# Attention terms earlier on GpSimd, first y ahead of K's transposes, near entries at level 5, x moved by two queues

## The chip, the cores and the metric

The kernel runs on one core of one Trainium2 chip. The metric is the device time of one execution in microseconds. The core has five engines that run their own instruction streams and meet at semaphores: TensorE (PE, matmuls and transposes), VectorE (DVE), ScalarE (ACT), GpSimd (POOL) and SyncE (SP), which here issues all transfers.

## The reference

Three layers in a row. The first is a gated linear attention over 768 time steps, 4 batches and 8 heads of 48 features; then a gated layer and an ELU layer on the 3072 tokens of 384 features.

```python
for t in range(S):
    cur = np.einsum('bhd,bhe->bhde', u[None] * kt, vt)
    y[:, :, t] = np.einsum('bhd,bhde->bhe', rt, state + cur)
    state = wt[:, :, :, None] * state + np.einsum('bhd,bhe->bhde', kt, vt)
...
gate = 1.0 / (1.0 + np.exp(-(x @ w_gate)));  val = x @ w_val
x = gate * val @ w_out
...
h = x @ w_in
g = np.where(h > 0.0, h, np.exp(np.minimum(h, 0.0)) - 1.0)
return g @ w_out
```

w_gate, w_val and w_out of the gated layer are (384, 1536), (384, 1536) and (1536, 384); the last layer's are (384, 2048) and (2048, 384).

## The kernel before

Time is cut into six blocks of 128 steps, each block into two halves of two batches: twelve half blocks, q = 0 to 11. For each, attention runs through the stages Tw, Tk, Tr (TensorE transposes w, k, r; ScalarE copies them out of PSUM), the levels L1 to L6, KT, Y and S, each stage in two parts b = 0 and 1 (one batch each).

The matrix A of scores between steps of a block is built by levels: at level li, runs of L = 2^li steps are paired. VectorE multiplies the later half of each pair of R by decays (`next_level_r`, L875; L879 at the last level), GpSimd the earlier half of K (`next_level_k`, L520), TensorE multiplies the two (L601, L607), and the result goes into A, by VectorE's predicated copies at L1 to L3 (L910), by ScalarE's copies at L4 to L6. The decays of all levels are products of neighbours (L952), made during the transposes by the table `DECAYS`.

The entries of A on the diagonal and one below it, the near entries, come from the untransposed inputs in `nat` (places 0, 1, 2 for r, k, w) and `shift` (r one step later): GpSimd multiplies r'k into `shift` (L498, at L1), rk into k's place of `nat` (L503, at L2) and that by u (L510, at L3); VectorE sums over features at L4 (L917, L921), combines the sums into `near` at L5, and at KT copies `near` into A under a mask (L937). Y multiplies A by V (L621) and adds the old state's part (L627); ScalarE copies it to yT, and SyncE moves it as ten transfers into xs, the input of the gated layer (`move_y`, L380). S updates the state. V, `nat` and `shift` of the next half block are loaded as ten transfers (`load_half`, L328; `load_v`, L349; `load_shift`, L339), once VectorE's sum over rk (d_shift) has freed `nat`.

The gated layer runs over seven sets of tokens: two of 256 columns (half blocks 0 and 1), then five of 512. A set is a list of groups, gate (g), value (v) and output (o) for each of 12 slices of w_gate, w_val and w_out, each in thirds. All products are made from high and low parts: ScalarE writes xh, hh and the weights' high parts, VectorE subtracts to get xl (L958), hl (L962) and the weights' low parts (L983); VectorE also makes h = sig * value (L973). The 36 pieces of these weights are loaded through a ring of four slots (`load_w1`; each load waits until the slot's last piece is split) and split in the first set, the first six ahead of it, in the steps of the list `EARLY`. Piece x = 12 is the first that is loaded after set 0 has begun.

`PROGRAM` is one list of steps, which TensorE, ScalarE and VectorE all walk in this order: half block 0 alone, then each set's thirds with the attention steps of later half blocks spread between them by shares. Set 0 runs beside half block 1, set 1 beside 2 and 3, and sets 2 to 5 beside pairs of half blocks, an even and an odd one; the last set and the ELU layer run without attention. SyncE and GpSimd have orders of their own: SyncE's is written out in its block, GpSimd walks the attention steps alone.

## Time and profile before

| | us |
|---|---|
| median of 3 runs | 1151.97 |
| the runs | 1151.76, 1151.97, 1169.11 |
| the profiled execution | 1157.96 |
| its span | 1156.2 |

| engine | busy us | share of the span |
|---|---|---|
| TensorE, matmuls | 1076.0 | 93% |
| TensorE, weight loads | 928.4 | 80% |
| VectorE | 630.5 | 55% |
| ScalarE | 482.9 | 42% |
| GpSimd | 255.5 | 22% |

The span is that of the profiled execution from the first instruction to the last; its time also holds what lies around it, 1.8 us. All times of instructions are from the start of the span. "L875" is a line of the kernel. In a row of the timeline, the bracket gives how long the engine had been idle and what ended that; a row with x2 or more merges instructions that followed each other.

### The profile page before, as it was taken

The page shows a single profiled execution, that of the slowest core. Times are in us where ns is not written, and L with a number is a line of the kernel's source. Part 1 is how long each engine was busy: PE and PEld are TensorE (multiplying, and loading weights), DVE is VectorE, ACT ScalarE, POOL GpSimd, SP SyncE. Part 2 cuts the span into 40 slices and gives each one's busy share as a digit, 9 for nine tenths or more (in the row PEclk, how much of TensorE's full clock was granted, in tenths as well). Part 3 has the DMA queues.
Part 4 walks back from the last instruction along what each step waited for, and adds up shares of the span by engine and source line. Part 5 has one row for each costly group of instructions (what it writes and reads, how often), then busy time and mean ns, then how long its engine had stood idle before and what let it go on. Part 6 is the DMA issues. An engine that isn't in the chain of part 4 may idle for free.

```text
span 1156.2 us, 19950 instructions
## 1 busy us (share of the span) xinstructions
PE 1076.0 (93%) x8124; PEld 928.4 (80%) x8124; DVE 630.5 (55%) x914; ACT 482.9 (42%) x871; POOL 255.5 (22%) x258
## 2 busy tenths in 40 slices
PE   5576798899999999999999999999999999999998
PEld 4576788877787778778777888889999998999998
DVE  6576778584939484947585633353434333343433
ACT  2434533434343334333433333464545444454543
POOL 8232155151606151524243300000000000000000
PEclk9888999999999999999999999999999999999999
DMA  6527130513413141404130041120101001010000
GB/s 123 104 64 141 51 63 16 90 21 56 63 42 41 37 63 42 59 18 62 42 62 15 9 143 55 55 83 1 55 1 56 1 17 39 1 55 1 28 1 28
DMA packets 154331, 54.97 MB, mean 48 GB/s; under 512 B 115968, under 2 KB 151936, under 8 KB 154240
## 3 DMA queue, kind: packets, MB, share of 16 engines
q1 hardware_dynamic: 154240, 53.70, 21.8%
q8 instruction: 65, 1.06, 0.4%
...
## 4 chain that ended last, share of the span: by engine, by line
PE 72%; DVE 15%; issue 5%; ACT 4%; SPq 2%; DMA 1%; DVEq 0%; ACTq 0%
PE ps L661 19%; PE ps L694 18%; PE ps L686 17%; PE ps L670 8%; DVE RKW L875 6%; DVE A L910 4%; PE ps L586 3%; ACT RKW L715 2%; PE ps L601 2%; PE ps L621 2%; PE ps L627 2%; DVE work L973 1%; DVE hl L962 1%; ACT hh L715 1%; SPq L380 1%
## 5 line engine op out<-in xcount | busy, mean ns | idle before, releaser
L661 PE MATMUL ps<-xh,WS 128*128 128x512 f32 (+1 forms) x1008 | 253.6, 371 | 16.4 <-DVE xl L958 12.0
L715 ACT ACTIVATE hh<-work 128x512 fp32r<-128x512 f32 (+1 forms) x180 | 108.8, 605 | 294.4 <-DVE work L973 209.7
L661 PEld LDWEIGHTS ps<-xh,WS 128*128 128x128 f32 x1008 | 173.4, 192 | 46.5 <-issue 7.3
L694 PE MATMUL ps<-WS,hh 128*128 128x384 f32 x768 | 197.7, 338 | 0.6 <-DVE hl L962 0.6
L670 PE MATMUL ps<-hh,WS 128*128 128x512 f32 (+1 forms) x504 | 162.0, 376 | 19.9 <-DVE hl L962 19.9
L962 DVE TENSOR_TENSOR hl<-work,hh 128x512 fp32r<-128x512 f32 (+1 forms) x180 | 125.6, 698 | 98.9 <-ACT hh L715 98.2
L686 PE MATMUL ps<-xh,WS 128*128 128x512 f32 x576 | 163.3, 396 | 0.0
L520 POOL TENSOR_TENSOR RKW<-RKW,WL 128x256 f32<-128x256 f32 x144 | 124.8, 880 | 158.2 <-PE ps L601 131.6
L1000 DVE SCALAR_TENSOR_TENSOR work<-work,ps 128x512 f32<-128x512 f32 x96 | 66.1, 688 | 168.2 <-ACT work L823 168.2
L694 PEld LDWEIGHTS ps<-WS,hh 128*128 128x128 f32 x768 | 140.7, 188 | 8.1 <-DVE hl L962 1.1
L661 PE MATMUL ps<-xl,WS 128*128 128x512 f32 (+1 forms) x504 | 133.0, 373 | 0.0
L694 PE MATMUL ps<-WS,hl 128*128 128x384 f32 x384 | 129.7, 338 | 0.0
L670 PEld LDWEIGHTS ps<-hh,WS 128*128 128x128 f32 x504 | 93.9, 193 | 38.5 <-DVE hl L962 23.4
L686 PEld LDWEIGHTS ps<-xh,WS 128*128 128x128 f32 x576 | 107.5, 189 | 18.2
L875 DVE TENSOR_TENSOR RKW<-RKW,WL 128x512 f32<-128x512 f32 x120 | 115.7, 982 | 5.7 <-PE ps L601 5.5
L601 PEld LDWEIGHTS ps<-RKW 128*64 128x64 f32 x1920 | 68.4, 145 | 50.1 <-DVE RKW L875 37.9
L601 PE MATMUL ps<-RKW 128*64 128x64 f32 x1920 | 81.4, 236 | 27.3 <-DVE RKW L875 26.5
L821 ACT ACTIVATE work<-ps 128x512 f32<-128x512 f32 x96 | 57.1, 595 | 111.9 <-PE ps L686 111.9
L661 PEld LDWEIGHTS ps<-xl,WS 128*128 128x128 f32 x504 | 86.4, 192 | 13.3
L670 PE MATMUL ps<-hl,WS 128*128 128x512 f32 (+1 forms) x252 | 91.7, 364 | 0.0
L973 DVE TENSOR_TENSOR work<-work,ps 128x512 f32<-128x512 f32 (+1 forms) x84 | 51.2, 609 | 73.0 <-PE ps L661 54.8
L781 ACT ACTIVATE work<-ps 128x512 f32<-128x512 f32 (+1 forms) x84 | 45.1, 537 | 105.0 <-PE ps L661 103.2
...
## 6 DMA issues: line engine op xcount, KB each, us to landing
...
```

The lines of the kernel that those rows point to most:

```text
L520: gp.tensor_tensor(Kb[:, :, :, 0, :], Kb[:, :, :, 0, :], Wb[:, :, :, 1].to_broadcast([P, PR, P // (2 * L), L]), ALU.mult).then_inc(p_k, 1)
L601: last = mm(bank[own, g * C:(g + 1) * C].rearrange("p (e i l) -> p e i l", e=2, l=L), K[:, g, own], Rb[:, :, :, 1, :], start=True, stop=True)
L661: last = mm(ps[:, VAL if val else GATE, t], gate_w(a, val, j, c), xp[b][:, c, t], start=(i == 0 and c == 0), stop=(i == 2 and c == KC - 1))
L670: last = mm(ps[:, ACC + i, t], down_w(a, j, i), hp[b][:, j % 2, t], start=(j == 0 and at == 0), stop=(j == F1 - 1 and at == 2))
L686: last = mm(ps[:, UP2 + j % 4, :], up2_w(a, j, c), xp[b][:, c, :], start=(i == 0 and c == 0), stop=(i == 2 and c == KC - 1))
L694: last = mm(ps[:, ACC2 + b, 0:HD], hp[ap][:, j % 2, b * P:(b + 1) * P], down2_w(wp, j), start=(j == 0 and i == 0), stop=(j == F2 - 1 and i ...
L715: return nc.scalar.activation(o, i, ACT.Copy)
L821: nc.scalar.activation(sig, ps[:, UP2 + j % 4, :], ACT.Relu, scale=-1.0).then_inc(a_relu, 1)
L875: last = tt(Rb, Rb, Wb.unsqueeze(1).unsqueeze(3).to_broadcast([P, 2, n, L]), ALU.mult)
L962: tt(hl[:, j % 2, t], h[:, t], f32(hh[:, j % 2, t]), ALU.subtract).then_inc(d_lo, 1)
L973: tt(h[:, t], sig[:, t], ps[:, VAL, t], ALU.mult).then_inc(d_h, 1)
L1000: nc.vector.scalar_tensor_tensor(h, sig, -1.0, ps[:, UP2 + j % 4, :], ALU.add, ALU.max).then_inc(d_elu, 1)
```

## The change

Five edits. GpSimd's products r'k and rk move from L1 and L2 to Tw, and u's from L3 to Tk; rk is written into w's place of `nat`, so it waits for Tw's transposes (half block 0 keeps the old places in the order). VectorE's sums move from L4 to Tk and Tr, the last decays from Tr to Tk; with the sum over rk at Tr, the loads of the next half block are freed there, and SyncE's order is changed accordingly. The near entries are copied into A at L5, for 32 partitions and 32 columns at a time, in place of KT. In half block 0 Y comes ahead of KT and S, and the six early w1 splits go to KT, S and the next Tw. The ten transfers of the first y are issued half by SyncE, half by ScalarE, and four w1 loads that stood ahead of them now stand behind.

```diff
+    FIRST = STAGES[:-3] + ["Y", "KT", "S"]
+    PARTS = [[("a", q, name, b) for name in (FIRST if q == 0 else STAGES) for b in range(U)] for q in range(NQ)]
...
-    EARLY = [("a", 0, name, b) for name in ("L5", "L6", "KT") for b in range(U)]
+    EARLY = [("a", q, name, b) for q, name in ((0, "KT"), (0, "S"), (1, "Tw")) for b in range(U)]
...
+                if q > 0:
+                    sp.wait_ge(s_att, count("a", q - 1, "Tr", 1))
                 wait(sp, d_shift, q)
...
+                for head in range(0, H, 2 if q == 0 else 1):
+                    for dst, src in y_pieces(q, head):
+                        sp.dma_start(dst, src).then_inc(xs_loaded, 16)
...
             load_shift(1)
+            move_y(0)
             load_w1(NR1 + ONCE, 2 * NR1 + ONCE)
-            move_y(0)
-            at = min(N1, NR1 + split_until(("a", 1, "L4", 1)))
-            load_w1(2 * NR1 + ONCE, at)
             load_half(2)
             load_v(2)
             load_shift(2)
-            load_w1(at, N1)
+            load_w1(2 * NR1 + ONCE, N1)
             move_y(1)
...
-                    if phase["a", q, "L4", 1] == m and q + 1 < NQ:
+                    if phase["a", q, "Tr", 1] == m and q + 1 < NQ:
...
                 elif part == "rk":
                     pool.wait_ge(nat_loaded[0], 32 * (q + 1))
-                    pool.wait_ge(p_shift, q + 1)
-                    gp.tensor_tensor(own, own, heads(nat[:, 0]), ALU.mult).then_inc(p_diag, 1)
+                    pool.wait_ge(nat_loaded[1], 32 * (q + 1))
+                    pool.wait_ge(s_att, count("a", q, "Tw", 1))
+                    gp.tensor_tensor(dest, own, heads(nat[:, 0]), ALU.mult).then_inc(p_diag, 1)
...
-            TERMS = {("L1", 1): "r'k", ("L2", 1): "rk", ("L3", 1): "u"}
+            FIRST_TERMS = {("L1", 1): ["r'k"], ("L2", 1): ["rk"], ("L3", 1): ["u"]}
+            TERMS = {("Tw", 1): ["r'k", "rk"], ("Tk", 0): ["u"]}
...
-                    pe.wait_ge(d_diag, 2 * q + b + 1)
+                    pe.wait_ge(d_diag, 4 * (q + 1))
...
                     copy(yT[:, b, :], ps[:, bank_of("a", q, name, b), :]).then_inc(a_y, 1)
+                    if q == 0 and b == 1:
+                        act.wait_ge(a_y, 2)
+                        for head in range(1, H, 2):
+                            for dst, src in y_pieces(q, head):
+                                nc.scalar.dma_start(dst, src).then_inc(xs_loaded, 16)
...
-            DECAYS = {("Tw", 1): [0], ("Tk", 0): [1], ("Tk", 1): [2, 3], ("Tr", 0): [4, 5, 6]}
+            DECAYS = {("Tw", 1): [0], ("Tk", 0): [1, 2, 3], ("Tk", 1): [4, 5, 6]}
...
+                    if name == f"L{NM + 1}" and b == 1:
+                        dve.wait_ge(a_score, (NL - NM) * q + 1)
+                        dve.wait_ge(d_mask, masked(q, NM - 1))
+                        dve.wait_ge(d_near, 2 * (q + 1))
+                        C = HP // 2
+                        for c in range(P // C):
+                            own, half = slice(c * C, (c + 1) * C), slice(c * C // 2, (c + 1) * C // 2)
+                            nc.vector.copy_predicated(
+                                A[own, :, :, own].rearrange("p g e (i j) -> p (g e) i j", j=2),
+                                masks[own, 0, half].bitcast(I32).unsqueeze(1).unsqueeze(3).to_broadcast([C, 2 * G, C // 2, 2]),
+                                near[own].unsqueeze(2).to_broadcast([C, 2 * G, C // 2, 2])).then_inc(d_diag, 1)
...
+                if (name, b) == (("L4", 0) if q == 0 else ("Tk", 1)):
+                    dve.wait_ge(p_shift, q + 1)
+                    nc.vector.reduce_sum(dots[:, :, 2], shift[:].rearrange("p g e d -> p (g e) d"), axis=AX.X
+                                         ).then_inc(d_dots, 1)
+                elif (name, b) == (("L4", 1) if q == 0 else ("Tr", 1)):
+                    dve.wait_ge(p_diag, 2 * (q + 1))
+                    nc.vector.reduce_sum(dots[:, :, 1], nat[:, 2].rearrange("p g (e d) -> p (g e) d", e=2)[:, :, 0:D],
+                                         axis=AX.X).then_inc(d_shift, 1)
```

VectorE from half block 0's last levels to the split of x. Before: WS rows are w1 low halves, L879 the last level's products, L937 the near copies, L947 the state's sum, L952 the decays, L958 xl.

```order
30 L983 TENSOR_TENSOR WS<-work,WS 128x384
31 L879 TENSOR_TENSOR RKW<-RKW,WL 64x4x64 x2
32 L983 TENSOR_TENSOR WS<-work,WS 128x384
33 L879 TENSOR_TENSOR RKW<-RKW,WL 64x4x64 x2
34 L983 TENSOR_TENSOR WS<-work,WS 128x384
35 L937 COPY_PREDICATED A<-masks,near 128x1024
36 L983 TENSOR_TENSOR WS<-work,WS 128x384
37 L937 COPY_PREDICATED A<-masks,near 128x1024
38 L983 TENSOR_TENSOR WS<-work,WS 128x384
39 L947 TENSOR_TENSOR ST<-SW,ps 48x8x48 x2
```

The same place in the change (line numbers are those of the changed kernel: L930 the near copies, L886 the last level's products, L994 w1 low halves, L950 the state's sum, L955 decays, L958 now the sum over shift, L969 xl):

```order
28 L930 COPY_PREDICATED A<-masks,near 32x16x32 x4
29 L886 TENSOR_TENSOR RKW<-RKW,WL 64x4x64 x4
30 L994 TENSOR_TENSOR WS<-work,WS 128x384 x3
31 L950 TENSOR_TENSOR ST<-SW,ps 48x8x48 x2
32 L994 TENSOR_TENSOR WS<-work,WS 128x384 x2
33 L955 TENSOR_TENSOR WL<-RKW 128x512
34 L994 TENSOR_TENSOR WS<-work,WS 128x384
...
40 L955 TENSOR_TENSOR WL<-WL 128x8
41 L958 TENSOR_REDUCE dots<-shift 128x16
42 L969 TENSOR_TENSOR xl<-xs,xh 128x256 x3
```

The near copies have gone ahead of the last level, the w1 low halves behind it and among the next half block's decays, and all seven decays and a sum now stand ahead of xl.

SyncE after the loads of half block 1. Before: four w1 loads, then the ten transfers of y to xs.

```order
19 L339 DMA shift<-in_r_dram 64x8x48 x2
20 L363 DMA work<-in_moe_w_out_dram 128x384
21 L359 DMA work<-in_moe_w_gate_dram 128x3x128
22 L359 DMA work<-in_moe_w_val_dram 128x3x128
23 L363 DMA work<-in_moe_w_out_dram 128x384
24 L380 DMA xs<-yT 48x2x128 x2
```

In the change (L388 the transfers of y, L371 and L375 w1 loads, L340 the loads of half block 2):

```order
19 L351 DMA shift<-in_r_dram 64x8x48 x2
20 L388 DMA xs<-yT 48x2x128
21 L388 DMA xs<-yT 32x2x128
22 L388 DMA xs<-yT 16x2x128
23 L388 DMA xs<-yT 48x2x128 x2
24 L375 DMA work<-in_moe_w_out_dram 128x384
25 L371 DMA work<-in_moe_w_gate_dram 128x3x128
26 L371 DMA work<-in_moe_w_val_dram 128x3x128
27 L375 DMA work<-in_moe_w_out_dram 128x384
28 L340 DMA nat<-in_w_dram 128x8x48 x2
```

Half of y's transfers are left, they stand ahead of the four w1 loads, and the loads of half block 2 follow right behind those, where 15 more w1 loads stood ahead of them.

GpSimd from the end of half block 1 on. Before (L538 the decayed state, L520 K's products):

```order
36 L538 TENSOR_TENSOR SW<-ST,WL 64x384 x2
37 L520 TENSOR_TENSOR RKW<-RKW 128x256 x2
38 L520 TENSOR_TENSOR RKW<-RKW,WL 128x128x2 x2
39 L498 TENSOR_TENSOR shift<-shift,nat 128x768
40 L520 TENSOR_TENSOR RKW<-RKW,WL 128x64x4 x2
41 L503 TENSOR_TENSOR nat<-nat 128x16x48
42 L520 TENSOR_TENSOR RKW<-RKW,WL 128x32x8 x2
43 L510 TENSOR_TENSOR nat<-nat,ub 128x8x48 x2
```

In the change (L540 and L522 for the same):

```order
37 L540 TENSOR_TENSOR SW<-ST,WL 64x384 x2
38 L498 TENSOR_TENSOR shift<-shift,nat 128x768
39 L503 TENSOR_TENSOR nat<-nat 128x16x48
40 L522 TENSOR_TENSOR RKW<-RKW 128x256
41 L510 TENSOR_TENSOR nat<-nat,ub 128x8x48 x2
42 L522 TENSOR_TENSOR RKW<-RKW 128x256
43 L522 TENSOR_TENSOR RKW<-RKW,WL 128x128x2 x2
```

r'k and rk are ahead of K's first product, u between its two parts, and the levels follow without them.

## Rows read from the trace of the kernel before

**Rows 1.** Busy time by stretch, all engines: stretch, busy, clock granted, DMA share, GB/s.
```profile
core 0: us, PE busy (x) PEld busy (x) DVE busy (x) ACT busy (x) POOL busy (x), PEclk, DMA share, GB/s
0.00:54.00 54.00, 29.32 (x336) 25.06 (x336) 35.34 (x57) 19.94 (x39) 31.47 (x40) 0.95 0.65 121
54.00:128.00 74.00, 55.14 (x579) 52.23 (x579) 49.18 (x82) 30.15 (x70) 18.04 (x18) 0.85 0.40 90
128.00:224.00 96.00, 81.19 (x1017) 75.41 (x1016) 70.95 (x110) 39.51 (x89) 40.22 (x40) 0.96 0.31 54
224.00:1156.00 932.00, 910.32 (x6196) 775.73 (x6196) 475.06 (x666) 393.25 (x674) 165.78 (x160) 1.00 0.17 39
```

**Rows 2.** Timeline, VectorE's near copy and TensorE's Y of half block 0.
```profile
37.13 1.29 DVE L937 COPY_PREDICATED A<-masks,near 128x1024 f32<-128x1024 int32 x1
...
38.57 1.95 PE L621 MATMUL ps<-A,V 128*48 128x128 f32 x16 [3.13 <-DVE A L937]
```

**Rows 3.** Timeline, from y's transfers to the first dense matmul.
```profile
44.45 6.54 SPq L380 DMA_DIRECT2D xs<-yT  x10
...
52.85 1.10 DVE L958 TENSOR_TENSOR xl<-xs,xh 128x256 fp32r<-128x256 f32 x3 [3.75 <-ACT xh L715]
...
54.10 0.98 PE L661 MATMUL ps<-xh,WS 128*128 128x256 f32 x3 [7.13 <-DVE xl L958]
```

**Rows 4.** Waits of TensorE, 54 to 128 us: total, times, longest.
```profile
PE ps L670 <- DVE hl L962: 14.0, 3, 6.5
...
PE ps L661 <- DVE WS L983: 2.3, 2, 1.2
```

**Rows 5.** Timeline, SyncE, ScalarE and TensorE about the longest wait.
```profile
98.50 0.99 SPq L328 DMA_DIRECT2D nat<-in_w_dram  x2
...
108.94 0.62 SPq L359 DMA_DIRECT2D work<-in_moe_w_gate_dram  x1
...
112.07 0.52 ACT L715 ACTIVATE WS<-work 128x384 fp32r<-128x384 f32 x1 [6.79 <-DMA work<-in_moe_w_gate_dram]
...
113.57 0.58 PE L670 MATMUL ps<-hh,WS 128*128 128x256 f32 x1 [6.47 <-DVE hl L962]
```

**Rows 6.** Timeline, VectorE and GpSimd at L1 and L2 of half block 1.
```profile
64.86 2.60 DVE L910 COPY_PREDICATED A<-masks,ps 64x512 f32<-64x512 int32 x2
...
74.83 1.00 DVE L983 TENSOR_TENSOR WS<-work,WS 128x384 fp32r<-128x384 f32 x1 [0.90 <-ACT WS L715]
...
75.38 2.20 POOL L503 TENSOR_TENSOR nat<-nat 128x768 f32<-128x768 f32 x1
...
75.76 2.96 DVE L875 TENSOR_TENSOR RKW<-RKW,WL 128x512 f32<-128x512 f32 x2
...
78.65 1.40 DVE L910 COPY_PREDICATED A<-masks,ps 64x512 f32<-64x512 int32 x2
```

**Rows 7.** One line, VectorE's level products: ns min, median, max, first and last start.
```profile
L875 DVE TENSOR_TENSOR RKW<-RKW,WL x120: 674/714/2361, 14.4 to 644.0; 128x512 f32<-128x512 f32 x120
```

**Rows 8.** Timeline of TensorE, gaps in a steady pair (L5 even, L1 odd).
```profile
479.58 0.69 PE L601 MATMUL ps<-RKW 128*64 128x64 f32 x16 [0.78 <-DVE RKW L875]
...
513.79 0.69 PE L601 MATMUL ps<-RKW 128*64 128x64 f32 x16 [1.94 <-DVE RKW L875]
```

**Rows 9.** Waits of TensorE, 128 to 224 us: total, times, longest.
```profile
PE ps L601 <- DVE RKW L875: 3.0, 7, 0.8
```

**Rows 10.** Timeline behind L5 and L6 of an even half block.
```profile
374.51 1.21 DVE L962 TENSOR_TENSOR hl<-work,hh 128x512 fp32r<-128x512 f32 x1
...
377.74 0.39 PE L670 MATMUL ps<-hh,WS 128*128 128x512 f32 x1
```

**Rows 11.** Timeline of TensorE, second part of Tw and L1, even half block.
```profile
450.37 0.60 PE L586 MATMUL ps<-ident,nat 128*128 128x128 f32 x4
...
459.62 1.39 PE L601 MATMUL ps<-RKW 128*64 128x64 f32 x32
```

**Rows 12.** Groups of GpSimd by form: count, busy us, mean ns, idle before.
```profile
L510 POOL TENSOR_TENSOR nat<-nat,ub 128x384 f32<-128x384 f32 x24 | 29.3, 1242 | 0.0
L503 POOL TENSOR_TENSOR nat<-nat 128x768 f32<-128x768 f32 x12 | 26.7, 2229 | 0.0
```

47 lines of the change are left out of this document (13 added, 34 removed).

## The prediction

> **What bounds the kernel now.** I read first the busy time by stretch [rows 1]. TensorE is idle for 24.7 us of the first 54, for 18.9 of the next 74, 14.8 of the next 96 and 21.7 of the 932 after that. From 630 us on attention is over and TensorE works without gaps; nothing in the change touches that part, so what it can win lies before. Then I asked the timeline what TensorE waited for at each gap, and looked at that engine in the same stretch.
>
> *Before 54 us* everything hangs on the first half block (q=0). The near entries are written into A by two predicated copies at KT, the first from 37.13 us, and Y starts at 38.57 after 3.13 us of waiting [rows 2]. From 44.45 SyncE issues ten transfers of y one after the other, 6.54 us, ScalarE and VectorE split x, and the first dense product starts at 54.10, after 7.13 us of idleness [rows 3].
>
> *54 to 128 us*: three waits for hl take 14.0 us, two for a low half of w1 2.3 [rows 4]. The longest is 6.47 us at 113.57. SyncE, which had waited for the rk sum at L4, issues the ten loads of the next half block from 98.50 to 108.90, and only then the next w1 piece, whose split starts at 112.07 [rows 5]; the two waits for a low half stand before and behind the same jam. The other two waits for hl (7.5 together), and one of 2.0 for h, follow level products of VectorE's that overlap GpSimd's: at L2 a pair takes 2.96 us while GpSimd's rk product of 2.20 runs [rows 6], where the median of one is 0.71 and the longest 2.36 [rows 7]. At L1 and L3 the pairs take 2.92 and 2.57.
>
> *224 to 630 us*: TensorE is idle for 17.9 us, nearly all of it in level matmuls (L601) that wait for VectorE's R product, in one pattern for each of the four pairs of half blocks: four waits in the even one, the last of them 0.78, 2.37 us together; one of 1.94 in the odd one [rows 8].
>
> **Part 1, the first half block: +1.5 us.** Without w1 splits in L5 and L6, VectorE ends L5's second product at about 31.8, and the near copies follow at once. Their form (32 partitions, 512 elements) isn't in the trace. Nearest are L2's copies of 512 elements at 0.70 each (1.40 for two) and L1's at 1.30 (2.60 for two) [rows 6]; by elements the old near copy, 1024 in 1.29 [rows 2], gives 0.65. I take 0.70, as all but L1's agree: four are 2.8 us, to 34.6; bounds 2.6 and 5.2. Y then starts at about 34.7 against 38.57, and yT is ready 3.9 us earlier, at 40.6. The ten transfers are shared: five on SyncE at 0.65 are 3.3 us, issued by 43.9; before they were by 50.99. That is 7 us on paper, and I count none of it, since ScalarE and VectorE aren't free then. The trace has no transfer issued by ScalarE: its price lies between nothing and, by SyncE's, 0.65; I take 0.65. ScalarE is then held until 43.9, and still has ahead of x the six evacuations of KT, Tw and Tk (0.60 each) and six w1 splits (0.52, as at 112.07 [rows 5]): 6.7 us, to 50.6. VectorE follows it with six low halves (0.55), the state's sum (1.14), seven decays (2.3) and, new here, the sum over shift (0.94): 7.7 us from 45.0, to 52.7. With S's matmuls and Tw's transposes, which both wait for ScalarE, I come to 53.6, and xl (1.10) ends at 54.7. GpSimd's rk and u products run in this stretch too, and hold VectorE's products beside them; I add 1 us, less than the 1.5 that the pair at 75.76 lost. So the first dense product starts at about 55.6: what the earlier Y gives is spent on splits that used to lie ahead of Y and now stand between Y and x. Bounds -2.5 (issues for nothing, no holding) to +4.
>
> What two issuing queues give, the rows leave open: they show only that SyncE's own issues don't overlap [rows 3]. The Trainium skill, "Perfetto Trace Analysis", section "DMA Instruction — HWDGE (DVE, Sync)", says that an issue locks a descriptor generator, which sequencers share, for exclusive use. By that rule ten issues take 6.5 us on two queues as well, ScalarE is held until 47.1, and this part is +4.7 instead of +1.5. No run here shows it.
>
> **Part 2, the loads of half block 2: -7.8 us.** They now wait for the rk sum at Tr. VectorE does it at about 62.5, SyncE is busy for 10.4 us until 72.9, then issues w1 piece 12, which is ready 3.1 us later (108.94 to 112.07 [rows 5]), at 76.0. Before, its low half ran at 74.83 [rows 6]; now it is due at about 75 on ScalarE. So a new wait of about 1 us takes the place of 6.5 + 2.3 = 8.8. After that SyncE has only w1 pieces until move_y(1). In later sets the loads just come earlier, and no wait of TensorE for them is in the trace: 0.
>
> **Part 3, VectorE at the levels, to 128 us: -2.1 us.** With GpSimd's three terms gone from L1 to L3, each pair there costs 1.4. At L1 the rk sum has moved in ahead (0.94), so 0.5 is left of 1.5; L2 gives 1.5, L3 1.2: 3.2 off waits of 9.5. Against it the near copies are one block of 2.8 us at L5, ahead of h, where groups of 256 columns need VectorE every 3 us: I put 1.5 there, less 0.4 that Y waited for them at 121.75.
>
> **Part 4, the clock: -1.5 us.** The granted clock is 0.85 over 54 to 128 and 0.96 over 128 to 224 [rows 1]: 11 and 4 us short of full clock, mostly around the waits themselves. With half of these gone I take a tenth of the 15 off; at most 4, at least nothing.
>
> **Part 5, half blocks 2 and 3, 128 to 224: -3.0 us.** Of 14.8 us idle [rows 1] 3.0 are levels waiting for R [rows 9], and about as much stands behind held products and near copies at Y: 5.6 go. Near blocks at L5 and the sum at Tr give back 2.6.
>
> **Part 6, the steady pairs: -6.6 us.** The even half block's 2.37 us stand behind held pairs at L2 and L3 and the two sums at L4, all of which leave: four times 2.37 is 9.4. The 1.94 of the odd one [rows 8] is the way from TensorE over ScalarE to VectorE at Tr, and stays. New are rk and u beside the decays. From Tw's end (450.97) to L1's start at 459.62 are 8.6 us [rows 11]; GpSimd needs 2.23 + 0.87 + 2 x 1.24 + 0.87 = 6.5 [rows 12], as r'k can run earlier, so K's products are in time by 2 us. VectorE has 3.6 us of work of its own there and 0.94 more, with up to 2 us of holding, in 6.8 us: I take 0.35 us late in each of 8 half blocks, 2.8. At L5 the near block puts hl's end off from 375.7 to at most 377.2, and TensorE wants it at 377.74 [rows 10]: 0.
>
> The Trainium skill, "SBUF — State Buffer", section "Who interferes with whom", speaks against this part: a VectorE instruction with two SBUF inputs contends with GpSimd's reads wherever they meet. The trace agrees where they meet now (2.96 instead of 1.4 [rows 6]). By it the decays are held in place of the level products, and parts 3, 5 and 6 could be nothing, -7.8 instead of -19.5; that is rival 2.
>
> **Sum.** 1.5 - 7.8 - 2.1 - 1.5 - 3.0 - 6.6 = -19.5 us. The profiled execution took 1157.96 (span 1156.2), 6 above the median 1151.97; the stalls that I count would sit in both, so I take the sum off the median: **1132 us**. The ends of this mechanism are about -33 and -2.
>
> **Rivals.** (1) *ScalarE's queue.* The ten issues exclude each other, and x comes 3.3 us later still. For it: ScalarE and VectorE have no slack ahead of x; against it: nothing but that the queues are two. 1136. (2) *The holding only moves.* rk and u meet decays, Tr products and hl instead, and parts 1, 2 and 4 alone remain: 1144. For it: the decays read SBUF as the level products do; against it: between Tw and Tr TensorE waits for nobody in the trace. (3) *Slower: near copies at L1's price.* At 1.30 the block at L5 is 5.2 us, 2.4 more. In steady halves hl then ends at 379.6 where TensorE wants it at 377.74 [rows 10]: 1.9 us eight times, 15; in the three early ones 2.4 each, 7: 1132 + 22 = 1154. It starts to cost from 0.85 us a copy. L1's copies write every other pair of elements, the near ones 32 in a row, so it is unlikely. (4) *The sum at Tr comes late*, behind u on GpSimd: loads start after 65 us, and piece 12 becomes a wait of 4 us or more. 1136. (5) *More falls away:* the queue before x is covered, clock and waits go with it. 1121.
>
> **Numbers.** Forecast 0.45; rivals 0.12, 0.20, 0.04, 0.07 and 0.12. Range 1118 to 1147. Two per cent, about what a measurement of this kernel can tell from no change, is 23 us, hence 1129: below it lie rival 5 and a little under half of the forecast, 0.33; slower by so much needs rival 3 and more, 0.02.
>
> **What would show it.** Y starts near 34.7, the first dense matmul between 54 and 57, with ScalarE and VectorE busy up to it; near copies of 0.70; the wait at 113.57 gone and a short one near 76 on piece 12; pairs of products at L1 to L3 at 1.4; in steady pairs the 1.94 stays and the other four go; decays held. Wrong would be a first dense matmul at 50 (then my queue is no bound), or L601's waits unchanged.

## The result and the profile after

| | before | after |
|---|---|---|
| median, us | 1155.65 (20 runs) | 1163.10 (20 runs) |
| lowest, highest | 1151.58, 1169.11 | 1159.07, 1169.11 |
| profiled execution | 1157.96 | 1163.65 |
| its span | 1156.2 | 1161.9 |

The change made the kernel slower by 0.56%: the ratio is 1.0056, with an interval of 1.0040 to 1.0072. The forecast was 1132, range 1118 to 1147. The median of before drifted with more runs from 1151.97 to 1155.65 (1156.3 to 1158.3 beside the experiments below), so ratios are the safer measure; the profiles are compared stretch by stretch.

Busy time by stretch after the change, as [rows 1] but for TensorE alone:
```profile
core 0: us, PE busy (x), PEclk, DMA share, GB/s
0.00:54.00 54.00, 30.91 (x336) 0.97 0.69 121
54.00:128.00 74.00, 56.98 (x583) 0.82 0.42 90
128.00:224.00 96.00, 81.92 (x989) 0.91 0.34 52
224.00:1156.00 932.00, 907.65 (x6205) 0.99 0.18 39
```
Every stretch behind 54 us has a lower granted clock than before, even the long last one. The waits of TensorE by releaser, 54 to 128 us and then 224 to 640 us, answer to [rows 4] and [rows 8]:
```profile
PE ps L663 <- DVE xl L969: 8.4, 1, 8.4
PE ps L672 <- DVE hl L973: 6.0, 4, 3.9
PE ps L663 <- DVE work L984: 4.2, 2, 3.0
...
PE ps L603 <- DVE RKW L882: 16.7, 12, 2.5
PE ps L672 <- DVE hl L973: 4.6, 8, 0.9
```
The jam of 6.47 us is gone, and the level matmuls (L603, L601 before) wait twelve times where they waited twenty (17.2 us in all, 224 to 630), yet for nearly the same sum. Fewer and longer waits, and a lower clock behind them: that is where the forecast for the steady pairs broke.

The path to the first dense matmul, from the timeline (answers to [rows 2, 3]):
```profile
31.57 4.15 DVE L930 COPY_PREDICATED A<-masks,near 32x512 f32<-32x512 int32 x4
...
35.87 1.95 PE L623 MATMUL ps<-A,V 128*48 128x128 f32 x16 [3.04 <-DVE A L930]
...
42.69 3.31 SPq L388 DMA_DIRECT2D xs<-yT  x5
...
42.69 3.60 ACTq L769 DMA_DIRECT2D xs<-yT  x5
46.34 0.60 ACT L717 ACTIVATE RKW<-ps 128x512 f32<-128x512 f32 x1 [3.68 <-issue]
...
46.99 0.56 PE L637 MATMUL ps<-V,RKW 128*48 128x48 f32 x16 [3.94 <-ACT RKW L717]
...
50.63 2.70 DVE L994 TENSOR_TENSOR WS<-work,WS 128x384 fp32r<-128x384 f32 x2
...
50.98 1.94 POOL L503 TENSOR_TENSOR nat<-nat 128x768 f32<-128x768 f32 x1 [6.59 <-PE ps L588]
...
52.82 1.04 ACT L717 ACTIVATE xh<-xs 128x256 fp32r<-128x256 f32 x3
...
54.33 4.11 DVE L955 TENSOR_TENSOR WL<-WL 128x256 f32<-128x256 f32 x6
...
58.36 0.94 DVE L958 TENSOR_REDUCE dots<-shift 128x16 f32<-128x768 f32 x1
59.22 1.09 DVE L969 TENSOR_TENSOR xl<-xs,xh 128x256 fp32r<-128x256 f32 x3
...
60.45 0.98 PE L663 MATMUL ps<-xh,WS 128*128 128x256 f32 x3 [8.43 <-DVE xl L969]
```
The first dense matmul runs at 60.45 against 54.10. ScalarE has x split at 53.9; VectorE needs until 60.3, behind low halves and decays that run beside GpSimd's products: two low halves in 2.70 beside rk, six decays in 4.11 beside u and K's products.

Set 0, the near block at L5 and the w1 piece that had waited for the jam [rows 5]:
```profile
103.94 0.37 SPq L371 DMA_DIRECT2D work<-in_moe_w_gate_dram  x1
...
105.90 4.16 DVE L930 COPY_PREDICATED A<-masks,near 32x512 f32<-32x512 int32 x4
...
110.57 1.01 PE L663 MATMUL ps<-xh,WS 128*128 128x256 f32 x3 [3.04 <-DVE work L984]
...
113.43 0.58 PE L672 MATMUL ps<-hh,WS 128*128 128x256 f32 x1 [0.57 <-DVE hl L973]
```
A steady pair after the change: the first decay beside rk, h (L984) behind the decays and ScalarE waiting for it, the waits of an even and an odd half block:
```profile
460.24 1.88 POOL L503 TENSOR_TENSOR nat<-nat 128x768 f32<-128x768 f32 x1 [23.64 <-PE ps L588]
...
460.74 1.93 DVE L955 TENSOR_TENSOR WL<-RKW 128x512 f32<-128x512 f32 x1 [3.51 <-ACT RKW L717]
462.71 2.25 DVE L955 TENSOR_TENSOR WL<-WL 128x256 f32<-128x256 f32 x3
...
464.88 0.68 DVE L984 TENSOR_TENSOR work<-work,ps 128x512 f32<-128x512 f32 x1
...
465.59 0.63 ACT L717 ACTIVATE hh<-work 128x512 fp32r<-128x512 f32 x1 [3.05 <-DVE work L984]
...
470.84 0.69 PE L603 MATMUL ps<-RKW 128*64 128x64 f32 x16 [1.43 <-DVE RKW L882]
...
498.58 0.51 PE L672 MATMUL ps<-hh,WS 128*128 128x512 f32 x1 [0.92 <-DVE hl L973]
...
523.29 0.69 PE L603 MATMUL ps<-RKW 128*64 128x64 f32 x16 [2.51 <-DVE RKW L882]
```

**A ledger.** SyncE stores the output of a set to x_scratch (L404; L397 before), which gives a mark for each. From first dense matmul to first dense matmul, then from mark to mark:

| stretch, us | before | after | difference |
|---|---|---|---|
| to the first dense matmul | 54.10 | 60.45 | +6.35 |
| set 0, to 144.03 / 145.76 | 89.93 | 85.31 | -4.62 |
| set 1, to the mark at 223.75 / 229.52 | 79.72 | 83.76 | +4.04 |
| four steady sets, to 674.95 / 687.08 | 451.20 | 457.56 | +6.36 |
| last set, to 760.21 / 772.03 | 85.26 | 84.95 | -0.31 |

That is +11.8 us at 760, where the spans differ by 5.7 alone. The rest is no work of the change: in before's profile the ELU layer ran 1.6% slower (last section), 6.1 us over its length.

The same stretches, read for how long TensorE was idle and how far the granted clock fell short of full. Shortfall is (1 - granted clock) times length, added up over pieces of 4 us; it is an upper bound of its price, since the clock is also low while TensorE stands. Each cell is idle / shortfall in us (the e kernels are those of the next section):

| | set 0 | set 1 | four steady sets |
|---|---|---|---|
| before | 23.8 / 12.5 | 9.7 / 1.8 | 18.2 / 0.0 |
| after | 15.6 / 14.2 | 11.5 / 5.1 | 21.1 / 6.8 |
| e1 | 16.4 / 9.6 | 11.6 / 5.1 | 21.1 / 3.4 |
| e4 | 14.3 / 6.7 | 9.6 / 3.2 | 18.3 / 1.7 |
| e5 | 17.1 / 6.9 | 11.6 / 6.7 | 17.4 / 6.9 |
| e6 | 16.8 / 7.5 | 11.8 / 5.2 | 9.4 / 3.4 |
| e8 | 15.9 / 8.9 | 9.8 / 3.4 | 10.2 / 0.0 |
| e10 | 16.3 / 13.4 | 12.1 / 7.6 | 13.1 / 6.8 |
| e12 | 16.4 / 8.8 | 12.0 / 8.3 | 9.4 / 1.7 |

From the first dense matmul on the change took 3.5 us off TensorE's idle time (51.7 to 48.2) and added 11.8 to the shortfall (14.3 to 26.1). Together that is 8.3, where the marks give 5.8 for these three stretches, since the shortfall is an upper bound. The shortfall also differs between profiles whose orders agree: after and e1 differ only in the first y's transfers, and are 4.6 apart in set 0 and 3.4 in the steady sets. So a difference of a few us in one set, from one profile each, is read by its idle time.

### The profile page after: what moved, and what is told of

Its sections match the earlier page's. It is cut to its first block, busy times and chain, and to the rows that moved or that the text cites. A ratio compares the mean times of both kernels' runs of the same rounds, so it can differ in the third digit from the quotient of the medians.

```text
span 1161.9 us, 19972 instructions
## 1 busy us (share of the span) xinstructions
PE 1080.4 (93%) x8124; PEld 934.5 (80%) x8124; DVE 663.2 (57%) x938; ACT 479.0 (41%) x871; POOL 248.0 (21%) x258
## 4 chain that ended last, share of the span: by engine, by line
PE 74%; DVE 16%; ACT 4%; issue 4%; SPq 1%; DMA 1%; ACTq 0%; DVEq 0%
PE ps L663 19%; PE ps L696 17%; PE ps L688 17%; PE ps L672 10%; PE ps L603 5%; DVE WL L955 4%; DVE RKW L882 2%; ACT RKW L717 2%; PE ps L623 2%; DVE A L930 2%; PE ps L629 2%; DVE work L984 2%; DVE RKW L886 1%; PE ps L588 1%; DVE hl L973 1%
## 5 line engine op out<-in xcount | busy, mean ns | idle before, releaser
L663 PE MATMUL ps<-xh,WS 128*128 128x512 f32 (+1 forms) x1008 | 258.5, 377 | 16.8 <-DVE xl L969 12.3
L663 PEld LDWEIGHTS ps<-xh,WS 128*128 128x128 f32 x1008 | 177.5, 197 | 47.1 <-issue 8.6
L672 PE MATMUL ps<-hh,WS 128*128 128x512 f32 (+1 forms) x504 | 164.0, 380 | 16.0 <-DVE hl L973 16.0
L522 POOL TENSOR_TENSOR RKW<-RKW,WL 128x256 f32<-128x256 f32 x144 | 122.8, 869 | 213.1 <-PE ps L603 188.9
L663 PE MATMUL ps<-xl,WS 128*128 128x512 f32 (+1 forms) x504 | 135.2, 378 | 0.0
L672 PEld LDWEIGHTS ps<-hh,WS 128*128 128x128 f32 x504 | 94.9, 195 | 36.8 <-DVE hl L973 21.6
L688 PEld LDWEIGHTS ps<-xh,WS 128*128 128x128 f32 x576 | 107.1, 188 | 16.9
L603 PEld LDWEIGHTS ps<-RKW 128*64 128x64 f32 x1920 | 68.8, 149 | 50.4 <-DVE RKW L882 39.3
L603 PE MATMUL ps<-RKW 128*64 128x64 f32 x1920 | 79.7, 238 | 30.0 <-DVE RKW L882 29.5
L882 DVE TENSOR_TENSOR RKW<-RKW,WL 128x512 f32<-128x512 f32 x120 | 94.4, 816 | 16.2 <-PE ps L603 15.7
L663 PEld LDWEIGHTS ps<-xl,WS 128*128 128x128 f32 x504 | 88.5, 197 | 13.7
L672 PE MATMUL ps<-hl,WS 128*128 128x512 f32 (+1 forms) x252 | 92.7, 368 | 0.0
L984 DVE TENSOR_TENSOR work<-work,ps 128x512 f32<-128x512 f32 (+1 forms) x84 | 51.2, 609 | 70.6 <-PE ps L663 50.2
L717 ACT ACTIVATE RKW<-ps 128x512 f32<-128x512 f32 (+1 forms) x120 | 70.0, 592 | 42.4 <-PE ps L588 37.9
```

The lines of the kernel that those rows point to most:

```text
L522: gp.tensor_tensor(Kb[:, :, :, 0, :], Kb[:, :, :, 0, :], Wb[:, :, :, 1].to_broadcast([P, PR, P // (2 * L), L]), ALU.mult).then_inc(p_k, 1)
L603: last = mm(bank[own, g * C:(g + 1) * C].rearrange("p (e i l) -> p e i l", e=2, l=L), K[:, g, own], Rb[:, :, :, 1, :], start=True, stop=True)
L663: last = mm(ps[:, VAL if val else GATE, t], gate_w(a, val, j, c), xp[b][:, c, t], start=(i == 0 and c == 0), stop=(i == 2 and c == KC - 1))
L672: last = mm(ps[:, ACC + i, t], down_w(a, j, i), hp[b][:, j % 2, t], start=(j == 0 and at == 0), stop=(j == F1 - 1 and at == 2))
L688: last = mm(ps[:, UP2 + j % 4, :], up2_w(a, j, c), xp[b][:, c, :], start=(i == 0 and c == 0), stop=(i == 2 and c == KC - 1))
L717: return nc.scalar.activation(o, i, ACT.Copy)
```

## The experiments

Each kernel is the changed one with its five edits under flags. NEW is the list of half blocks whose products, sums and next loads are moved; NEAR5 that of those with near copies at L5; DECAYS_AT is the table of the decays. These are the values of before (-) and of the change (+):

```diff
-NEW = ()
-NEAR5 = ()
-DECAYS_AT = {("Tw", 1): [0], ("Tk", 0): [1], ("Tk", 1): [2, 3], ("Tr", 0): [4, 5, 6]}
-Y_FIRST = False
-EARLY_AT = ((0, "L5"), (0, "L6"), (0, "KT"))
-TWO_QUEUES = False
+NEW = range(1, 12)
+NEAR5 = range(12)
+DECAYS_AT = {("Tw", 1): [0], ("Tk", 0): [1, 2, 3], ("Tk", 1): [4, 5, 6]}
+Y_FIRST = True
+EARLY_AT = ((0, "KT"), (0, "S"), (1, "Tw"))
+TWO_QUEUES = True
```

In their profiles the changed kernel's lines stand 11 to 21 further down: L614 is its L603, L674 its L663, L683 its L672, L893 its L882, L974 its L955, L988 its L969. All in one table; "first" is the first dense matmul, "y to first" the way to it from the first transfer of y, "steady" the sum of the four steady stretches, "760" the mark after the last set, which is free of what the ELU layer does:

| | NEW | decays | NEAR5 | Y first | queues | first | y to first | set 0 | set 1 | steady | 760 | median | ratio to before (95%) |
|---|---|---|---|---|---|---|---|---|---|---|---|---|---|
| before | none | old | none | no | 1 | 54.10 | 9.65 | 89.9 | 79.7 | 451.2 | 760.2 | 1155.65 | |
| after | all | new | all | yes | 2 | 60.45 | 17.76 | 85.3 | 83.8 | 457.6 | 772.0 | 1163.10 | 1.0056 (1.0040-1.0072) |
| e1 | all | new | all | yes | 1 | 57.66 | 13.25 | 83.3 | 83.9 | 454.9 | 764.7 | 1157.89 | 0.9990 (0.9967-1.0014) |
| e2 | none | new | all | yes | 2 | 56.75 | 13.95 | 89.3 | 82.9 | 451.0 | 765.0 | 1158.24 | 0.9995 (0.9966-1.0023) |
| e3 | all | new | all | yes, old splits | 2 | 61.46 | 16.89 | 83.4 | 84.9 | 456.6 | 771.3 | 1162.29 | 1.0039 (1.0012-1.0067) |
| e4 | 1 | old | none | no | 1 | 55.44 | 9.63 | 78.2 | 81.0 | 452.8 | 752.3 | 1151.26 | 0.9912 (0.9880-0.9944) |
| e5 | all | new | 0 | yes | 2 | 59.38 | 17.78 | 82.1 | 84.9 | 453.0 | 764.3 | 1156.86 | 1.0003 (0.9973-1.0033) |
| e6 | all | old | none | no | 1 | 54.18 | 9.63 | 82.0 | 82.8 | 441.9 | 745.8 | 1138.31 | 0.9833 (0.9784-0.9881) |
| e7 | 1 | old | 4-11 | no | 1 | 55.34 | 9.63 | 77.8 | 79.6 | 454.2 | 751.9 | 1147.84 | 0.9909 (0.9879-0.9940) |
| e8 | all, cut | new | all | yes | 2 | 60.42 | 17.76 | 81.7 | 80.8 | 440.7 | 748.5 | 1140.13 | 0.9848 (0.9799-0.9897) |
| e9 | none | new | none | no | 1 | 56.80 | 9.62 | 90.3 | 79.0 | 450.7 | 761.7 | 1153.35 | 0.9981 (0.9962-0.9999) |
| e10 | all | old | all | yes | 2 | 58.03 | 16.49 | 85.0 | 86.1 | 449.9 | 763.9 | 1155.39 | 1.0003 (0.9978-1.0028) |
| e11 | 1, 4-11 | old | none | no | 1 | 54.06 | 9.63 | 78.6 | 80.3 | 441.7 | 739.7 | 1133.62 | 0.9812 (0.9782-0.9843) |
| e12 | all | old | 0 | yes | 1 | 56.16 | 11.99 | 82.3 | 86.7 | 440.5 | 750.6 | 1140.45 | 0.9867 (0.9842-0.9891) |

How far a "first" can be read: e4, e6, e7 and e11 do the same things in the same order up to there, and it was 55.44, 54.18, 55.34 and 54.06. And the near copies of half block 0 began at 31.57 in the changed kernel's profile and at 33.18 in e1's, though the two orders don't differ ahead of them. So differences of "first" under 1.5 us say nothing, and larger ones may hold 1.6 us of this. "y to first" is free of it: 9.62 to 9.65 in the six kernels without Y first, 17.76 to 17.78 in after, e5 and e8.

### e1: one queue

```diff
-TWO_QUEUES = True
+TWO_QUEUES = False
```


> The changed kernel with all ten transfers of the first y issued by SyncE again. In the changed kernel's profile ScalarE issues five of them from 42.69 to 46.29 us, KT's first evacuation starts at 46.34 and the first dense matmul at 60.45. Theory A (ScalarE held by its issues delays everything behind): KT's evacuation at about 42.8 us, first dense matmul at about 56.9, 3.6 earlier, though x lands at about 51 instead of 48. Rival B (VectorE's queue ahead of xl, stretched by GpSimd's rk and u products, sets the start): first dense matmul at 59.5 or later. The rest of the profile as in the changed kernel.

K's first transposes and the state's matmuls, which waited 3.94 us for ScalarE in the changed kernel:
```profile
43.68 1.09 PE L599 MATMUL ps<-ident,RKW 128*128 128x128 f32 x8
45.02 0.56 PE L648 MATMUL ps<-V,RKW 128*48 128x48 f32 x16 [0.25 <-ACT RKW L728]
...
57.66 0.98 PE L674 MATMUL ps<-xh,WS 128*128 128x256 f32 x3 [7.56 <-DVE xl L988]
```
SyncE alone took 6.51 us for ten, and the first dense matmul still came 2.8 us earlier, although y was ready 1.7 us later here (the transfers start at 44.41, not 42.69); the way from y's transfers to it is 4.5 us shorter. So the second queue gives x nothing that is used and holds up ScalarE, which has the evacuations and splits to do. The ratio to before fell from 1.0056 to 0.9990. The 2.0 us of set 0 and the 2.7 of the steady sets are not the queue's: TensorE's idle time there is no shorter, and only the clock's shortfall is smaller.

### e2: the products and sums as before

```diff
-NEW = range(1, 12)
+NEW = ()
```


> The changed kernel with GpSimd's three products, VectorE's two sums and the place of the next loads back at L1 to L4 (the decays stay at Tw and Tk, near copies at L5, Y first, two queues). Theory A (in the steady sets the holding only moved: a decay takes 1.85 us beside rk, and TensorE waits 1.4 and 2.5 us at L1): sets of 512 columns take 112.5 us or less again (changed kernel 112.5 to 115.1, kernel before 112.3), the first dense matmul comes 3 to 4 us earlier than 60.45, and the wait of 6 us for w1 pieces at L4 of half block 1 is back. Rival B (the block of four near copies at L5 is what costs): sets stay at 114 us or more.

The first dense matmul comes 3.7 us earlier (56.75; the way from y's transfers is 3.8 us shorter), set 0 is back at 89.3 with its jam, and the last three steady sets go to 111.9 each. So the moved products do cost in this surrounding, at the head and in steady sets, and win in set 0.

### e3: the early splits as before

```diff
-EARLY_AT = ((0, "KT"), (0, "S"), (1, "Tw"))
+EARLY_AT = ((0, "L5"), (0, "L6"), (0, "KT"))
```


> The changed kernel with the six early w1 splits back at L5, L6 and KT (KT now behind Y). Theory A (the splits that stand between Y and x are paid for there): first dense matmul about 2 us earlier than 60.45, at 58.5, Y at most 1 us later than 35.87. Rival B (VectorE and ScalarE would wait for TensorE anyway at these places): first dense matmul at 60 or later.

First dense matmul at 61.46, and Y starts at 37.84 instead of 35.87. Most of that delay isn't the splits': the near copies began at 33.53 here, and at 33.18 in e1, where the splits stand as in the change. From y's transfers on the way is 0.9 us shorter (16.89 against 17.76), where theory A had 2. So the place of the splits is worth less than 1 us while Y is first and two queues move it.

### e4: before, with half block 1 alone moved

```diff
-NEW = ()
+NEW = (1,)
```


> The kernel before with one edit, for half block 1 alone: its three products at Tw and Tk, its two sums at Tk and Tr, and the loads of half block 2 right behind. Theory A (in set 0 the gain is the jam of the loads that goes, at the price of a later start): first dense matmul at 55 to 56 instead of 54.10, the 6.47 us wait at L4 gone, and set 0 from its first dense matmul to that of set 1 about 83.5 us instead of 89.9; later sets as before (112.3); time 4 to 5 us under the kernel before. Rival B (the earlier loads jam w1 piece 12 in turn, and set 0's gain in the changed kernel came from near copies and splits): set 0 not under 88 us, time as before.

Set 0 took 78.2 us, 11.8 less than before and 7.1 less than after. The jam is gone, and the two other waits for hl are 3.51 and 1.60 where they were 4.87 and 2.69 (the 14.0 of [rows 4] less 6.47), as parts 2 and 3 said. Of the 11.8 us TensorE's idle time gives 9.5; the clock's shortfall fell as well, from 12.5 to 6.7. The time is 0.9% under before's.

### e5: near copies back at KT, but for half block 0

```diff
-NEAR5 = range(12)
+NEAR5 = (0,)
```


> The changed kernel with the near entries written as before (two copies of 128 partitions at KT) from the second half block on; all else as changed. Theory: in set 0 the four copies of about 1.04 us at L5 (4.16) delay h by 3.04 and what follows, and cost more than the 0.4 that Y used to wait: set 0, from its first dense matmul to that of set 1, falls from 85.3 to 80 to 82 us, the time falls by 2.5 to 5 us against the changed kernel, and steady sets grow by 0.4 (the run without the moved products showed 111.9 a set against 112.3). Rival: the near copies only show a delay that the moved products make, and set 0 stays at 84 to 86.

Set 0 fell by 3.2 us to 82.1 (1.2 under that of e1, though). But TensorE was idle there for 17.1 us against 15.6: the waits of 3.04 and 0.57 went, and one of 3.20 for a w1 piece at 112.40 came in their place. What fell is the clock's shortfall (6.9 against 14.2), so a cost of the near block in set 0 isn't shown. The last three steady sets stayed at 112.7, 0.2 over those of e1, with 3.7 us less of idleness over the four and 3.5 more of shortfall. The near block isn't what keeps the steady sets slow.

### e6: before, with all products, sums and loads moved

```diff
-NEW = ()
+NEW = range(1, 12)
```


> The kernel before with one part of the change alone: GpSimd's products, VectorE's two sums and the next loads at Tw, Tk and Tr from the second half block on. Theory: set 0 is as with only the second half block moved (78.2 us), set 1 pays about 3 for a wait at L1 of the third half block (as the 3.03 at 137.19) and 2 more for one in the first steady set; steady sets 112.5 to 113. In all -3 to -5 us against before, so 1 to 3 slower than the kernel with only the second half block moved. Rival: the moved products cost nothing when the near copies and the decays stay as before, and the time is 1144 to 1151.

Both were wrong, by far: 1138.3, 1.7% faster. The last three steady sets took 109.2 us; the first took 114.3 as before, with 2.2 us less of idleness and 3.4 of shortfall. Waits of TensorE over the steady sets, h in an even half block, and the wait of an odd one; they answer to [rows 8]:
```profile
PE ps L614 <- DVE RKW L893: 8.7, 4, 2.2
...
PE ps L683 <- DVE hl L992: 0.5, 3, 0.2
...
443.75 1.93 DVE L974 TENSOR_TENSOR WL<-RKW 128x512 f32<-128x512 f32 x1 [3.51 <-ACT RKW L728]
...
446.41 0.69 DVE L1003 TENSOR_TENSOR work<-work,ps 128x512 f32<-128x512 f32 x1 [0.27 <-PE ps L674]
...
447.13 0.63 ACT L728 ACTIVATE hh<-work 128x512 fp32r<-128x512 f32 x1 [1.58 <-DVE work L1003]
...
503.03 0.69 PE L614 MATMUL ps<-RKW 128*64 128x64 f32 x16 [2.17 <-DVE RKW L893]
```
17.2 us have become 8.7: all waits of even half blocks are gone, and one remains per pair, 2.17 instead of 1.94. Part 6 had 9.4 for the waits that go, and took off 2.8 for lateness that is new; 8.5 came. This kernel differs from the changed kernel in the decays, the near copies and the first half block.

### e7: near copies at L5 in steady half blocks alone

```diff
-NEW = ()
+NEW = (1,)
-NEAR5 = ()
+NEAR5 = range(4, 12)
```


> The kernel before with the products, sums and next loads of the second half block alone moved, and the near entries per 32 rows at L5 in the steady half blocks alone. Theory: set 0 78.2 us, steady sets 111.9 in place of 112.3, first steady set at most 115.9: 1 to 2 us under the run without the near part (median 1151.3, ratio 0.991), ratio to before 0.988 to 0.993. Rival: the 111.9 came from another part (the decays or Y first), and steady sets stay at 112.3.

The rival was right: the last two steady sets took 112.36 and 112.38, against 112.26 and 112.34 in e4. With products at L1 to L3 the near block's place is worth nothing.

### e8: the changed kernel with GpSimd's rk and u cut short

```diff
-                    gp.tensor_tensor(dest, own, heads(nat[:, 0]), ALU.mult).then_inc(p_diag, 1)
+                    few = slice(0, 1) if q > 1 else slice(None)
+                    gp.tensor_tensor(dest[:, few], own[:, few], heads(nat[:, 0])[:, few], ALU.mult).then_inc(p_diag, 1)
...
-                        mine = dest[:, b * H:(b + 1) * H, :]
+                        n = 1 if q > 1 else H
+                        mine = dest[:, b * H:b * H + n, :]
```
From half block 2 on, rk is made for one of its sixteen groups of 48 columns and u for one of eight in each part (the 24 in the text below is a slip); the sums are then made of what lies there.

> The changed kernel with the rk and u products of the third and later half blocks cut to one head of 24 (left out: the other heads' products, so dots are wrong there). The waits, sums and order stay. Theory (holding): decay 0 goes from 1.85 back to about 0.7 us, the waits of TensorE at L1 for the R product (3.03 at 137, 2.51 in odd steady half blocks, 1.43 in even ones) fall by 1 to 1.5 each or go, steady sets 110.5 to 111.8, the time 5 to 9 us under the changed kernel. Rival (queue): the waits come from VectorE's added work between Tw and L1 (the sum over shift, decays in another place) and from the way over ScalarE; steady sets stay within 0.3 of 112.5.

The last three steady sets took 109.7, 17 us less over the four (TensorE's idle time fell by 10.9, the clock's shortfall from 6.8 to 0.0), and the time was 1140.1. What VectorE's decays took in the steady sets (ns min/median/max), in the changed kernel, in e8 and in e6, one row each:
```profile
L955 DVE TENSOR_TENSOR WL<-WL x48: 166/586/1067, 234.8 to 630.9; 128x256 f32<-128x256 f32 x8, 128x128 f32<-128x128 f32 x8, 128x64 f32<-128x64 f32 x8, 128x32 f32<-128x32 f32 x8
```
```profile
L976 DVE TENSOR_TENSOR WL<-WL x48: 166/208/759, 226.9 to 608.2; 128x256 f32<-128x256 f32 x8, 128x128 f32<-128x128 f32 x8, 128x64 f32<-128x64 f32 x8, 128x32 f32<-128x32 f32 x8
L976 DVE TENSOR_TENSOR WL<-RKW x8: 692/693/693, 226.2 to 605.0; 128x512 f32<-128x512 f32 x8
```
```profile
L974 DVE TENSOR_TENSOR WL<-WL x48: 166/306/1069, 225.8 to 608.8; 128x256 f32<-128x256 f32 x8, 128x128 f32<-128x128 f32 x8, 128x64 f32<-128x64 f32 x8, 128x32 f32<-128x32 f32 x8
L974 DVE TENSOR_TENSOR WL<-RKW x8: 1750/1848/1934, 223.9 to 601.6; 128x512 f32<-128x512 f32 x8
```
The instructions are the same. Alone the six small decays have a median of 208 ns; in the changed kernel 586. In e6 the first decay is as much held as in the changed kernel (1848 against 1847, 693 alone), but the small ones are at 306. So the holding in itself isn't fatal; it matters how many decays stand beside the products.

### e9: before, with the decays alone moved

```diff
-DECAYS_AT = {("Tw", 1): [0], ("Tk", 0): [1], ("Tk", 1): [2, 3], ("Tr", 0): [4, 5, 6]}
+DECAYS_AT = {("Tw", 1): [0], ("Tk", 0): [1, 2, 3], ("Tk", 1): [4, 5, 6]}
```


> The kernel before with one part of the change alone: the seven decays one step earlier (1 to 3 at Tk of the first pairs, 4 to 6 at Tk of the second, none at Tr). Products, sums, near copies and the first half block as before. Theory (the decays' place costs only where GpSimd's rk and u products hold them): with the products still at L1 to L3 little changes, steady sets 111.9 to 112.4, the time within 3 us of before. Rival (their place costs by itself, since VectorE then has all seven ahead of the first product): steady sets 113 or more, the time 4 us or more over before.

The last three steady sets took 111.8, a gain of 0.5 each, and the first 115.4, a loss of 1.1; ratio 0.998, with an interval that ends at 0.9999. Alone the decays' move is a small gain at most: the wait of odd half blocks at L1 is 1.43 instead of 1.94.

### e10: the changed kernel with the decays of before

```diff
-DECAYS_AT = {("Tw", 1): [0], ("Tk", 0): [1, 2, 3], ("Tk", 1): [4, 5, 6]}
+DECAYS_AT = {("Tw", 1): [0], ("Tk", 0): [1], ("Tk", 1): [2, 3], ("Tr", 0): [4, 5, 6]}
```


> The changed kernel with the decays at their places of before, all else as changed. Theory (products moved and decays moved clash): the 2.51 and 1.43 at L1 in steady half blocks fall to 2.2 and about 0, steady sets 108.8 to 109.7 in place of 112.5 to 115, the 3.03 at L1 of half block 2 falls to about 1.5; the time 13 to 19 us under the changed kernel, 1144 to 1150. The first dense matmul moves by less than 2 from 60.45. Rival (near copies at L5 or the first half block's order cost it): steady sets stay over 111.5.

Half of it came: the 1.43 of even half blocks and one of the two waits of odd ones went, and the steady sum fell by 7.7 us to 449.9. But the sets behind the first were at 112.0, 111.9 and 110.5, not 109. Two neighbouring stretches of e10 about its wait of 2.17, then the same of e6:
```profile
512.56:520.56 8.00, 5.83 (x53) 0.96 0.03 5
520.56:528.56 8.00, 8.00 (x84) 0.83 1.31 170
```
```profile
498.46:506.46 8.00, 5.83 (x54) 1.00 0.18 37
506.46:514.46 8.00, 8.00 (x99) 1.00 1.23 161
```
The same wait, but in e10 the granted clock falls to 0.96 and 0.83 behind it: 8 us x 0.04 + 8 us x 0.17 = 1.7 us. With the wait for hl of 0.92, 24 us ahead of it, that makes 2.6 of the 2.7 that this set is longer than e6's. Near block and moved products together therefore do cost; each without the other didn't (e6, e7). Over the four sets e12, which has neither the near block past half block 0 nor the second queue and is otherwise e10, was idle for 9.4 us where e10 was idle for 13.1.

### e11: the best of these

```diff
-NEW = ()
+NEW = (1, *range(4, 12))
```


> The kernel before with the products, sums and next loads moved in half blocks 1 and 4 to 11 (0, 2 and 3 as before), decays and near copies as before. Theory: set 0 as with half block 1 alone (78.2), set 1's stretch to the first store ends near 215, then 114.3 and three times 109.2: 3 to 5 us under the run with all moved (1138.3), 1133 to 1136. Rival: the set with the change of pattern pays what is saved, and the time stays at 1137 to 1140.

1133.6, ratio 0.981: set 0 as in e4 (78.6 against 78.2) and the steady sets of e6. With the third half block's products left at L1 to L3, its L1 begins with a wait of 0.29 instead of e6's 1.27 and 1.75.

### e12: e6 with Y first

```diff
-NEAR5 = ()
-Y_FIRST = False
-EARLY_AT = ((0, "L5"), (0, "L6"), (0, "KT"))
+NEAR5 = (0,)
+Y_FIRST = True
+EARLY_AT = ((0, "KT"), (0, "S"), (1, "Tw"))
```


> The run with all products moved (1138.3) and, in the first half block, Y ahead of KT and S, with the early dense steps moved as in the change and the near entries of that half block at L5; one queue moves y, decays as before. Theory (Y first gives time that splits take back): the first dense matmul at 54 to 57 against 54.18, the time 1137 to 1141, no gain. Rival (Y first gains where nothing else holds VectorE): the first dense matmul at 50 to 53, the time 1134 to 1137. Against both: at 58 or later the first half block's order is what costs the changed kernel its 6 us there.

```profile
44.17 6.51 SPq L395 DMA_DIRECT2D xs<-yT  x10
...
52.11 1.03 ACT L728 ACTIVATE xh<-xs 128x256 fp32r<-128x256 f32 x3 [1.80 <-DMA xs<-yT]
...
56.16 0.98 PE L674 MATMUL ps<-xh,WS 128*128 128x256 f32 x3 [6.55 <-DVE xl L988]
```
y's transfers start only 0.3 us earlier than before's 44.45 (the near copies began at 33.16, late as in e1), the way from there is 11.99 us instead of 9.65, and the first dense matmul comes 2 us later. Had they started at 42.7, as in the changed kernel, it would have come at about 54.7, by an estimate from these numbers. The theory held: no gain.

## Why the prediction was wrong

*Part 6, the steady pairs (-6.6; measured +6.4).* This is the step that failed, and the sum with it. I had costed the decays beside rk and u as "up to 2 us of holding" with 0.35 us of it on the path of each half block, 2.8 in all. That leaves 10.6 us of waits at the levels (four times 1.94, and 2.8); they came to 16.7. The near block, put at 0, added 4.1 at hl, and the clock's shortfall, in no term, rose from 0.0 to 6.8. The two moves that meet here can now be told apart. The moved products and sums do what I said: e6 gains 9.3 us over the four sets, and its waits at the levels are 8.5 shorter. The diff also packed all decays ahead of L1, into the very steps to which rk and u went, and that I took as a harmless part: with NEAR5 empty or (0,), new decays cost nothing with the old products (e9, 450.7) and 11 to 13 us with the new (e5, 453.0 against e6, 441.9, and against e12, 440.5, which differs in the decays and the queue alone). e8, with the products cut, removes 16.9 us and leaves every order and wait as it is, so GpSimd's work beside the packed decays is the cause; neither of the two alone is. Its price came in two forms. Waits per pair: 1.43 and 0.22 + 2.51 at L1 instead of 2.17 alone. The way there leads over h and ScalarE: in the even half block h (L984) starts 4.14 us after the first decay, behind three more, in e6 2.66 us after it, behind one more. ScalarE waits 3.05 for it instead of 1.58 (lines in the result and at e6), and R's evacuations stand behind that in its order; those 1.47 us are close to the wait of 1.43 that follows. And the clock, which I took off as a gain of part 4 and nowhere as a loss. In the last steady set of the changed kernel it fell this far behind the wait of 2.5 at L1:
```profile
627.97:635.97 8.00, 5.24 (x43) 0.93 0.00 0
635.97:643.97 8.00, 8.00 (x64) 0.64 0.00 0
```
That is 8 x 0.07 + 8 x 0.36 = 3.4 us in one set, which took 115.1 where e1 and e3, with the same waits, took 112.5. So this part of the loss comes in some executions and not in others.

*Rival 2* had the right mechanism ("the holding only moves") and the wrong floor: it let parts 3, 5 and 6 be nothing, 1144. The held instructions were not worth the same in their new place. At L2 a held product delays one pair; ahead of L1 a row of held decays delays h and, over ScalarE, the start of the whole level. The rule of the Trainium skill that I weighed there ("SBUF — State Buffer", "Who interferes with whom") agrees with the traces once more: the first decay takes 1847 ns beside rk and 693 where rk is cut.

*The near block: "At L5 ... 0".* I put its copies at 0.70. They took 1.04 at the head and in set 0 (4.15 and 4.16 for four), with GpSimd's product of the next level beside them, and 0.82 in the steady half blocks (3.28 to 3.30 for four); the median of all 48 was 0.73. By my own bound a cost began at 0.85 a copy, and still TensorE waited 0.92 for hl at 498.58, which part 6 had ruled out. The bound left out what the block does to the last level's four products behind it: they ran beside GpSimd's products for the state and r'k and took 4.26 us, 2.91 in e6. In set 0 it showed as 3.04 + 0.57 where I had put 1.5. Rival 3 named this place, at 1.30 a copy and 1.9 us a half block, twice what came.

*Part 1 (+1.5, bounds to +4; measured +6.35).* Y started at 35.87, not 34.7, for the copies' price, and yT was ready at 42.67, not 40.6. ScalarE's five issues took 3.60 us, 0.72 each where I had 0.65, and stood in front of K's evacuation as I had it. What I mis-sized is VectorE's work between that and xl: 7.7 us in my sum and 1 added for holding, 11.7 in the trace (47.5 to 59.2). Of the 4.0 between 7.7 and 11.7, 1.6 are two low halves held beside rk and 2.5 the seven decays, at 4.8 where I had 2.3; in before's own trace they took 3.3 (0.69, 2.04 and 0.60), so 2.3 was a wrong reading too. The runs price the parts by the way from y's transfers to the first dense matmul, which the change made 8.1 us longer: one queue takes off 4.5 (e1), products as before 3.8 (e2), decays as before 1.3 (e10), splits as before 0.9 (e3). These overlap and can't be added. And the queue question: both queues issued at the same time, five in 3.31 and five in 3.60, where one issued ten in 6.5. They don't exclude each other here, and rival 1 falls. The Trainium skill, "Perfetto Trace Analysis", "DMA Instruction — HWDGE (DVE, Sync)", names DVE and Sync as the sequencers that share the locked generator; I had stretched that to ScalarE. It did not matter, since ScalarE's time was the scarce thing, not SyncE's.

*Parts 2 and 3 (-7.8 and -2.1).* Right in mechanism: the jam is gone, pairs of products are at 1.28 at L1 and L2 and at 1.74 at L3. The short wait near 76 on piece 12 did not come. Clean, in e4, set 0 is 11.8 us shorter, where the two parts had 9.9. In the changed kernel it gave -4.6: TensorE's idle time fell by 8.2, near the forecast, but the clock's shortfall rose by 1.7, where it fell by 5.8 in e4.

*Part 4 (-1.5)* was wrong in sign: the granted clock was 0.82 over 54 to 128 and 0.91 over 128 to 224, 0.85 and 0.96 before. Together with the steady sets this is the largest change of all in the profile: 11.8 us more shortfall (3.8 in e1).

*Part 5 (-3.0; measured +4.0).* L1 of half blocks 2 and 3 begins with waits of 3.03 and 3.38, and hl is waited for 2.16 behind the near block. Here the decays aren't at fault: with their old places the first is 1.27 + 1.75 (e6), as long. That sets whose groups have 256 columns leave too little room for the products between Tw and L1 is my guess, and no run took it apart. Leaving these two half blocks as they were is worth 2.5 us in set 1 and 3.4 in set 0 (e11 against e6).

*What stays open.* With half block 2's products moved, a w1 piece is waited for 3.20 us in e5, e6 and e12 and 1.6 in e4, e7 and e11; I didn't trace that to its end. Why the clock falls behind one wait of 2.17 and not behind another is open too: e10 differs from e6 in the 0.92 us of idleness before, but after, e1 and e3 have the same steady orders and waits and shortfalls of 6.8, 3.4 and 5.2 us.
